# Reordering the products of a gated linear attention among GpSimd, VectorE and the schedule's slots, in a fused attention, low-rank mix and two-FFN kernel

## The chip, the cores and the metric

The kernel runs on one core of a Trainium2 chip. The time is that of one execution on the device, in microseconds (us); lower is better. All operands are float32; matmul operands of the feed-forward parts are split into a rounded part ("hi") and a remainder ("lo").

## The reference

The input has 4 batches, 8 heads, 768 tokens and head size 48.

```
f = sigmoid(f_logit)                       # attention with a gated state
state = f[t][:, None] * state + outer(k[t], v[t])
y[t] = q[t] @ state
x = y, heads side by side                  # 4 x 768 x 384
u = x + (x.T @ U @ V).T                    # low-rank mix over tokens, rank 32
x = u + relu(u @ w_ch1) @ w_ch2            # 384 -> 1536 -> 384
h = relu(x @ w_in)                         # 384 -> 1024
c = 3-tap convolution of h over tokens, by channel
out = (h * sigmoid(c)) @ w_out             # 1024 -> 384
```

## The kernel before

**Work.** Tokens go in units of 128; two units are a duo, so a batch is 3 duos and the whole input is duos 0 to 11 (`NDUO`). The attention of a duo is a list of steps (`STEPS`): `EVEN`, levels 0 to 5, `T`, `U`, `Y`. Within chunks of 64 tokens the products of gates are built by doubling. `EVEN` makes each token's own product of q and k (`blocks<-q_t,k_t`, L1031), multiplies the even tokens of q by their gates on VectorE (L1034) and then those of k on GpSimd (L1187, `k_t<-k_t,gates`), after which GpSimd makes the products of pairs of gates (L1190). At a level TensorE makes 64 small matmuls of q and k (L595). Then VectorE multiplies half of q by the gate products (L1041 at level 0, L1052 above), copies the scores that belong to the level from PSUM under a mask (`take_scores`, L988 and L994), and from level 2 on makes the products for the next level (`blocks<-blocks`, L1059, "the merge"); GpSimd multiplies half of k (L1187, `k_t<-k_t,blocks`) and at level 1 also makes the next products (L1190). The next level's matmuls wait for q, for k and for the scores taken. `T` transposes k on TensorE (L605), `U` updates the states (L617, with L1011 to L1022 on VectorE), `Y` makes the output y (L641).

**Feed-forward.** After attention a batch has a low-rank sum (`rank`: L679 on TensorE, L1085 and L1088 on VectorE), its split in three parts of 32 rows in `rstack` (`rank_split`: three ScalarE copies L882, one VectorE subtraction L1093) and the mix (L690, L697). Then come 24 slots of the first feed-forward part (`first1`, L712 to L714; `second1`, L731 to L736, two slots later) and 16 slots of the second (`first2`, L751 to L753; `second2`, L770 to L775, three slots later). In a slot q of `first2` ScalarE applies the relu (L916), VectorE makes the convolution in three instructions (L1131 and two L1134), ScalarE the sigmoid (L903), VectorE the product with h (`mul2`, L1118), ScalarE the rounded part (L909) and GpSimd the remainder (`lo2`, L1224). The convolution of slot q writes one of two buffers and waits for `lo2` of slot q - 2. At `x2_split` GpSimd makes a remainder of the input of the second part (L1218).

**Order.** One list, `ORDER`, made by `schedule()`, holds all tasks; each engine runs its own part of each task in that order, in its own queue, and waits on semaphores. Duos 0 to 2 run ahead of all feed-forward work. The steps of duos 3(b+1) to 3(b+1)+2 are laid into the slots of batch b: slot numbers go from 0 to 39, with one level per slot in `first1` and one in two slots in `first2`. In each slot the order is: in batch 0 two weight pieces (`piece`: a load issued by SyncE, a rounding copy by ScalarE L875, a remainder by GpSimd L1197), the first matmuls, the attention step, the second matmuls, `whole`, `x2_split` (GpSimd), `second2`, `split2` (which holds `lo2` of the slot before).

The step `EVEN` of a batch's first duo stands in slot 0 of the batch in which it runs, and that of the others one slot before level 0.

Of the kernel before, what the change touches and what calls it, by code (L numbers as in the profile page):

```python
# [68 lines left out]
def schedule():  # L69
# [17 lines left out]
    for b in range(B):  # L87
# [5 lines left out]
        if b + 1 < B:  # L93
            n = DUOS * (b + 1)
            for j in range(DUOS):
                for i, st in enumerate(STEPS):
                    s = (len(STEPS) + 1) * j + i + (st == Y and j < DUOS - 1)
                    if b == 0:
                        s -= 2
                        if s < 0:  # L100
                            continue

                    s = s if s < 2 * N1 else 2 * s - 2 * N1
                    at.setdefault(s, []).append((n + j, st))
        left = list(range(FIRST + 3, len(PIECES))) if b == 0 else []
        for s in range(2 * N1 + 2 * N2):
            if s < 2 * N1:
                order += [("piece", left.pop(0)) for _ in range(2) if left]
                order.append(("first1", b, s))
                if s < 2:  # L110
                    order += [("mix", b, CT + i) for i in ([0], [1, 2])[s]]
            else:
                order += [("states", n) for n, st in at.get(s - 1, []) if st == U]
                order.append(("first2", b, s - 2 * N1))
            if s < 2 * N1:
                order += [("states", n) for n, st in at.get(s - 1, []) if st == U]
            for n, st in at.get(s, []):
                order.append(("att", n, st))
                if st == U and n + 1 < NDUO:
                    order.append(("gates", n + 1))  # L120
            q = s - LAG1
            if 0 <= q < 2 * N1:
                order.append(("second1", b, q))
                if q % N1 == N1 - 1:
                    order.append(("x2", b, q // N1))
            if s in WHOLE_SLOTS:
                order.append(("whole", b, WHOLE_SLOTS.index(s)))
            for part in range(2):
                i = s - LAG1 - N1 * (part + 1)
                if 0 <= i < CT:  # L130
                    order.append(("x2_split", b, part, i))
            q = s - 2 * N1 - LAG2
            if b + 1 < B and s == 2 * N1 + 2 * N2 - 1:
                order += [("rank", b + 1, j) for j in range(DUOS)]
            if q >= 0:
                order.append(("second2", b, q))
                if q % N2 == N2 - 1:
                    order.append(("out", b, q // N2))
            if s > 2 * N1:
                order.append(("split2", b, s - 2 * N1 - 1))  # L140
# [47 lines left out]
def taken(n, st):  # L188

    return TAKEN_AT["att", n, st]  # L190
# [117 lines left out]
def bass_gla_lowrank_mix_ffn_gated_conv_ffn(nc, qT, kT, fT, qn, kn, vn, vp, mix_u, mix_v, w_ch1, w_ch2,  # L308
                                            w_in, conv_w, w_out, mask_in, ident_in, out):
    with ExitStack() as ctx:  # L310
# [83 lines left out]
        carried, y_done = sem("carried"), sem("y_done")  # L394
        x_copied, x_copied_last = sem("x_copied"), sem("x_copied_last")
        rank_done, rank_summed = sem("rank_done"), sem("rank_summed")
        rank_hi_ready, rank_ready = sem("rank_hi_ready"), sem("rank_ready")
        mix_done, u_hi_ready, u_lo_ready = sem("mix_done"), sem("u_hi_ready"), sem("u_lo_ready")
        ff1_done, r_hi_ready, r_lo_ready = sem("ff1_done"), sem("r_hi_ready"), sem("r_lo_ready")
        second_done = sem("second_done")  # L400
# [156 lines left out]
        def _(pe):  # L557
# [124 lines left out]
            def mix_task(b, i):  # L682
# [9 lines left out]
                first, width = units[0] * P, (CUT if part == 0 else HALF)  # L692
                if i == 0:
                    pe.wait_ge(rank_ready, b + 1)
                    pe.wait_ge(rank_hi_ready, 3 * (b + 1))
                    pe.wait_ge(vstack_ready, 1)
                pe.matmul(o[:, 0:width], rstack[:, t * P:(t + 1) * P], vstack[:, first:first + width],  # L697
                          start=False, stop=True, skip_group_check=True).then_inc(mix_done, 1)
# [99 lines left out]
        def _(act):  # L798
# [78 lines left out]
            def rank_split(b):  # L877
                act.wait_ge(rank_summed, 3 * (b + 1))
                if b > 0:
                    act.wait_ge(mix_done, 2 * CT * b)  # L880
                for i in (2, 0, 1):
                    nc.scalar.copy(rstack[RANK * i:RANK * (i + 1), :], rank_sum[:]).then_inc(rank_hi_ready, 1)  # L882

            def mix_task(b, i):
# [77 lines left out]
        def _(dve):  # L962
# [61 lines left out]
            def attention(n, st):  # L1024
# [21 lines left out]
                elif st < LEVELS:  # L1046
# [4 lines left out]
                    view = split_blocks(q, c)[:, :, 1, :]  # L1051
                    nc.vector.tensor_tensor(view, view, block_product(products(gates[i], blocks[i], st), c, 0),  # L1052
                                            ALU.mult).then_inc(q_ready, 1)
                    if by_vector(n, st):
                        dve.wait_ge(level_taken, taken(n, st - 1))
                        take_scores(n, st)
                    if st >= 2:
                        pairs = products(gates[i], blocks[i], st).rearrange("p (n two) -> p n two", two=2)
                        nc.vector.tensor_tensor(products(gates[i], blocks[i], st + 1), pairs[:, :, 0], pairs[:, :, 1],  # L1059
                                                ALU.mult).then_inc(merged_ready, 1)  # L1060
                elif st == T and n == 0:
                    dve.wait_ge(vstack_hi, 1)
                    lo = slice(RANK, 2 * RANK)
# [13 lines left out]
            def rank_task(b, j):  # L1077
# [2 lines left out]
                dve.wait_ge(rank_done, UNITS * (b + 1))  # L1080
                if b > 0:
                    dve.wait_ge(rank_ready, b)
                    dve.wait_ge(rank_hi_ready, 3 * b)
                sums = [ring_bank(ring_use(b, "rank", 0), DM)[RANK * i:RANK * (i + 1), :] for i in range(3)]
                nc.vector.tensor_copy(rank_sum[:], sums[0]).then_inc(rank_summed, 1)  # L1085
                for i in (1, 2):
# [1 line left out]
                    nc.vector.tensor_tensor(rank_sum[:], sums[i], rank_sum[:], ALU.add).then_inc(rank_summed, 1)  # L1088

            def rank_split(b):  # L1090
                dve.wait_ge(rank_hi_ready, 3 * b + 1)
                lo = slice(2 * RANK, 3 * RANK)
                nc.vector.tensor_tensor(rstack[lo, :], rank_sum[:], rstack[lo, :], ALU.subtract).then_inc(rank_ready, 1)  # L1093

# [69 lines left out]
        def _(pool):  # L1164
# [5 lines left out]
            def attention(n, st):  # L1170
# [9 lines left out]

                    pool.wait_ge(q_ready, scaled(n, EVEN))
                else:
                    pool.wait_ge(level_done, levels(n, st))
                    pool.wait_ge(k_ready, gated(n, st - 1))
                    products_made(pool, n, st)
                view = split_blocks(k, c)[:, :, 0, :]
# [102 lines left out]
```

## Time and profile before

| what | value |
|---|---|
| time, median of 3 runs | 724.39 us (724.3 to 727.32) |
| time of the profiled execution | 722.35 us |
| its span in the profile | 720.5 us |
| TensorE matmul busy | 683.1 us, 95% |
| VectorE busy | 430.1 us, 60% |
| GpSimd busy | 282.6 us, 39% |
| ScalarE busy | 251.0 us, 35% |

The span is what the trace covers; the profiled execution's own time is 1.85 us longer. A busy share is the union of an engine's instruction times over the span, and an instruction's time includes what it spends held up once it has started. PE is the matmul side of TensorE, DVE is VectorE, ACT ScalarE, POOL GpSimd.

### The profile page before, as it was taken

The numbers are of one execution on the slowest core, as the hardware profiler recorded it, in microseconds if no ns is written. First come the engines' busy times: TensorE is split into PE (matmuls) and PEld (weight loads), VectorE is DVE, ScalarE is ACT, GpSimd is POOL, SyncE is SP. The second block draws the span as 40 slices with busy tenths as digits, with TensorE's granted clock in tenths as the row PEclk, the third lists the DMA queues.
The fourth block names the chain that finished last, engine by engine and source line by source line (L and its number), as shares of the span: only waits on it lengthen the run. The fifth ranks groups of instructions, "written<-read, shape, count | busy, mean of one in ns | idle before, by whom it ended". The sixth has DMA issues, their size and how long they took to land.

```text
span 720.5 us, 22499 instructions
## 1 busy us (share of the span) xinstructions
PE 683.1 (95%) x10076; PEld 644.5 (89%) x10076; DVE 430.1 (60%) x721; ACT 251.0 (35%) x512; POOL 282.6 (39%) x262
## 2 busy tenths in 40 slices
PE   2897899999999999999999999999999999999998
PEld 1786788998999989999999889989999989999997
DVE  6895753754787664364597765265389751122875
ACT  1044534251255512113245431312144551121553
POOL 4872774883442243152263235045154221030432
PEclk9999999999999999999999999999999999999999
DMA  8331544322002010200201110211000100000000
GB/s 206 92 92 37 146 135 115 95 78 67 3 23 79 26 32 24 61 9 25 67 2 56 46 57 3 59 32 25 24 2 2 35 34 1 0 1 1 1 34 33
DMA packets 22720, 33.47 MB, mean 46 GB/s; under 512 B 3584, under 2 KB 15616, under 8 KB 22624
## 3 DMA queue, kind: packets, MB, share of 16 engines
q1 hardware_dynamic: 21616, 30.27, 15.0%
q10 hardware_dynamic: 1008, 1.77, 1.0%
q8 instruction: 79, 1.29, 0.8%
q14 instruction: 17, 0.14, 0.1%
HBM read 27.31 MB, written 4.72 MB: 44 GB/s over the span
## 4 chain that ended last, share of the span: by engine, by line
PE 86%; DVE 5%; POOL 4%; issue 3%; ACT 2%; DMA 1%; ACTq 0%; DVEq 0%; POOLq 0%
PE acc L731 8%; PE att L595 8%; PE acc L732 7%; PE acc L736 6%; PE hb L712 6%; PE hb L713 6%; PE hb L714 6%; PE acc L770 5%; PE hb L751 5%; PE hb L753 5%; PE hb L752 5%; PE acc L771 5%; PE acc L775 5%; PE att L641 3%; POOL k_t L1187 3%
## 5 line engine op out<-in xcount | busy, mean ns | idle before, releaser
L1104 DVE SCALAR_TENSOR_TENSOR r_lo<-hb,r_hi 128x386 fp32r<-128x386 f32 (+1 forms) x96 | 53.5, 558 | 195.3 <-ACT r_hi L894 195.2
L894 ACT ACTIVATE r_hi<-hb 128x386 fp32r<-128x386 f32 (+1 forms) x96 | 47.2, 492 | 256.5 <-PE hb L714 256.5
L1224 POOL TENSOR_TENSOR r_lo<-conv,r_hi 128x384 fp32r<-128x384 f32 x64 | 63.7, 995 | 147.3 <-ACT r_hi L909 147.3
L1187 POOL TENSOR_TENSOR k_t<-k_t,blocks 112x512 f32<-112x512 f32 x60 | 81.7, 1364 | 89.9 <-PE att L595 81.0
L731 PE MATMUL acc<-r_hi,w_ch_hi 128*128 128x386 f32 (+1 forms) x288 | 103.1, 358 | 0.0
L712 PE MATMUL hb<-u_hi,w_ch_hi 128*128 128x386 f32 (+1 forms) x288 | 98.2, 341 | 0.2 <-DVE r_lo L1104 0.2
L713 PE MATMUL hb<-u_hi,w_ch_lo 128*128 128x386 f32 (+1 forms) x288 | 97.6, 339 | 0.0
L732 PE MATMUL acc<-r_hi,w_ch_lo 128*128 128x386 f32 (+1 forms) x288 | 97.3, 338 | 0.0
L714 PE MATMUL hb<-u_lo,w_ch_hi 128*128 128x386 f32 (+1 forms) x288 | 96.9, 337 | 0.0
L595 PEld LDWEIGHTS att<-q_t,k_t 48*64 48x64 f32 (+3 forms) x3840 | 58.7, 134 | 28.9 <-issue 16.8
L1134 DVE SCALAR_TENSOR_TENSOR conv<-hb,convw,conv 128x384 f32<-128x384 f32 x128 | 79.1, 618 | 4.5
L595 PE MATMUL att<-q_t,k_t 48*64 48x32 f32 (+3 forms) x3840 | 65.3, 219 | 12.2 <-POOL k_t L1187 6.9
L1187 POOL TENSOR_TENSOR k_t<-k_t,gates 112x512 f32<-112x512 f32 x12 | 18.4, 1536 | 123.6 <-DVE q_t L1034 123.6
L770 PE MATMUL acc<-w_out_hi,r_hi 128*128 128x384 f32 x192 | 66.6, 347 | 0.0
L736 PE MATMUL acc<-r_lo,w_ch_hi 128*128 128x386 f32 (+1 forms) x288 | 66.0, 337 | 0.0
L751 PE MATMUL hb<-u_hi,w_in_hi 128*128 128x388 f32 x192 | 65.4, 341 | 0.0
L753 PE MATMUL hb<-u_lo,w_in_hi 128*128 128x388 f32 x192 | 65.0, 338 | 0.0
L752 PE MATMUL hb<-u_hi,w_in_lo 128*128 128x388 f32 x192 | 64.8, 338 | 0.0
L771 PE MATMUL acc<-w_out_lo,r_hi 128*128 128x384 f32 x192 | 64.7, 337 | 0.0
L1052 DVE TENSOR_TENSOR q_t<-q_t,blocks 112x512 f32<-112x512 f32 x60 | 60.1, 1002 | 4.1 <-PE att L595 2.4
L903 ACT ACTIVATE conv<-conv 128x384 f32<-128x384 f32 x64 | 33.7, 526 | 77.1 <-DVE conv L1134 77.1
L731 PEld LDWEIGHTS acc<-r_hi,w_ch_hi 128*128 128x128 f32 x288 | 54.2, 188 | 2.2
(140 smaller groups left out, 1295.9 us busy)
## 6 DMA issues: line engine op xcount, KB each, us to landing
v_p<-in_vn_dram SPq DMA_DIRECT2D x12, 384.0 KB, 3.6
out_dram<-ostage SPq DMA_DIRECT2D x24, 192.0 KB, 2.1
q_t<-in_qT_dram SPq DMA_DIRECT2D x21, 192.0 KB, 3.5
k_t<-in_kT_dram SPq DMA_DIRECT2D x21, 192.0 KB, 3.3
gates<-in_fT_dram SPq DMA_DIRECT2D x21, 192.0 KB, 3.5
ostage<-in_w_ch_dram SPq DMA_DIRECT2D x14, 192.0 KB, 2.9
conv<-in_w_ch_dram SPq DMA_DIRECT2D x10, 192.0 KB, 2.8
ostage<-in_w_out_dram SPq DMA_DIRECT2D x5, 192.0 KB, 2.5
```

The lines of the kernel that those rows point to most:

```text
L595: mm = pe.matmul(banks[o:o + left, par, g * C + half:g * C + half + 32], k[rows, first:first + left], moving, start=True, stop=True, skip_ ...
L712: pe.matmul(o, wh[:, t, ws], u_hi[:, t, cols], start=(t == 0), stop=False)
L713: pe.matmul(o, wl[:, t, ws], u_hi[:, t, cols], start=False, stop=False)
L714: mm = pe.matmul(o, wh[:, t, ws], u_lo[:, t, cols], start=False, stop=(t == CT - 1))
L731: pe.matmul(o, wh[:, j, ws], r_hi[:, s, 0:width], start=(j == 0), stop=False)
L732: pe.matmul(o, wl[:, j, ws], r_hi[:, s, 0:width], start=False, stop=False)
L736: mm = pe.matmul(o, wh[:, j, ws], r_lo[:, s, 0:width], start=False, stop=(j == N1 - 1))
L751: pe.matmul(o, wh[:, t, ws], u_hi[:, t, cols], start=(t == 0), stop=False)
L752: pe.matmul(o, wl[:, t, ws], u_hi[:, t, cols], start=False, stop=False)
L753: mm = pe.matmul(o, wh[:, t, ws], u_lo[:, t, cols], start=False, stop=(t == CT - 1))
L770: pe.matmul(o, r_hi[:, s, ts], wh[:, j, :], start=(j == 0), stop=False)
L1187: nc.gpsimd.tensor_tensor(view, view, block_product(ends, c, 1), ALU.mult).then_inc(k_ready, 1)
```

## The change

The edit has five parts.

1. GpSimd's product of k at a level no longer waits for the level's matmuls alone. At level 1 it waits for VectorE's product of q of this level, and at levels 2 to 5 for VectorE's merge.
2. On VectorE the merge goes ahead of the masked copy.
3. The step `EVEN` of a duo goes one slot earlier, next to `Y` of the duo before; that of the first duos of batches 2 and 3 (duos 6 and 9) goes from slot 0 of the batch in which it ran to slot 38 of the one before. Duo 3's stays.
4. The two weight pieces of a slot go from ahead of the first matmuls to behind the attention step.
5. In the split of the low-rank sum the middle rows are copied by VectorE instead of ScalarE, with a semaphore of their own.

```diff
@@ schedule() @@
-                    s = (len(STEPS) + 1) * j + i + (st == Y and j < DUOS - 1)
+                    s = (len(STEPS) + 1) * j + i + (st == Y and j < DUOS - 1) - (st == EVEN)
                     if b == 0:
                         s -= 2
-                        if s < 0:
-                            continue
+                    if s < 0:
+                        continue
...
+            if b + 2 < B:
+                at.setdefault(2 * N1 + 2 * N2 - 2, []).append((n + DUOS, EVEN))
         left = list(range(FIRST + 3, len(PIECES))) if b == 0 else []
         for s in range(2 * N1 + 2 * N2):
             if s < 2 * N1:
-                order += [("piece", left.pop(0)) for _ in range(2) if left]
                 order.append(("first1", b, s))
...
                     order.append(("gates", n + 1))
+            order += [("piece", left.pop(0)) for _ in range(2) if left]
             q = s - LAG1
@@ scalar, rank_split @@
-                for i in (2, 0, 1):
+                for i in (2, 0):
                     nc.scalar.copy(rstack[RANK * i:RANK * (i + 1), :], rank_sum[:]).then_inc(rank_hi_ready, 1)
@@ vector, attention, levels 1 to 5 @@
-                    if by_vector(n, st):
-                        dve.wait_ge(level_taken, taken(n, st - 1))
-                        take_scores(n, st)
                     if st >= 2:
                         pairs = products(gates[i], blocks[i], st).rearrange("p (n two) -> p n two", two=2)
                         nc.vector.tensor_tensor(products(gates[i], blocks[i], st + 1), pairs[:, :, 0], pairs[:, :, 1],
                                                 ALU.mult).then_inc(merged_ready, 1)
+                    if by_vector(n, st):
+                        dve.wait_ge(level_taken, taken(n, st - 1))
+                        take_scores(n, st)
@@ vector, rank_split @@
-                dve.wait_ge(rank_hi_ready, 3 * b + 1)
+                dve.wait_ge(rank_summed, 3 * b + 3)
+                if b > 0:
+                    dve.wait_ge(mix_done, 2 * CT * b)
+                nc.vector.tensor_copy(rstack[RANK:2 * RANK, :], rank_sum[:]).then_inc(rank_mid_ready, 1)
+                dve.wait_ge(rank_hi_ready, 2 * b + 1)
@@ gpsimd, attention @@
-                    pool.wait_ge(level_done, levels(n, st))
+                    if st == 1:
+                        pool.wait_ge(q_ready, scaled(n, st))
+                    else:
+                        pool.wait_ge(merged_ready, merged(n, st))
                     pool.wait_ge(k_ready, gated(n, st - 1))
```

The waits of TensorE's mix and of VectorE's rank sum on `rank_hi_ready` are split in two to match.

## Rows read from the trace of the kernel before

**Rows 1.** windows: us, busy us and count of each engine, granted clock, DMA share, GB/s

```profile
76.00:80.00 4.00, 2.58 (x12) 2.46 (x12) 3.32 (x5) 3.58 (x8) 2.06 (x3) 0.67 0.39 81
245.00:415.00 170.00, 167.61 (x2525) 157.27 (x2524) 103.95 (x178) 57.73 (x116) 58.71 (x52) 1.00 0.13 37
```

**Rows 2.** waits of PE, 80 to 585 us: us in total, times, longest

```profile
PE att L595 <- POOL k_t L1187: 4.3, 8, 1.0
```

**Rows 3.** timeline, 252 to 257 and 276 to 278 us: start, duration, engine, line, operation, idle before

```profile
252.97 0.68 DVE L1031 TENSOR_TENSOR blocks<-q_t,k_t 112x512 f32<-112x512 f32 x1
...
254.53 1.50 POOL L1187 TENSOR_TENSOR k_t<-k_t,gates 112x512 f32<-112x512 f32 x1 [6.94 <-DVE q_t L1034]
...
255.99 1.04 POOL L1190 TENSOR_TENSOR blocks<-gates 112x512 f32<-112x512 f32 x1
...
256.08 1.14 PE L595 MATMUL att<-q_t,k_t 48*64 48x32 f32 x64 [0.93 <-POOL k_t L1187]
...
276.87 0.76 PE L595 MATMUL att<-q_t,k_t 48*32 48x32 f32 x64
```

**Rows 4.** source view of L1187: count, duration min/median/max in ns

```profile
L1187 POOL TENSOR_TENSOR k_t<-k_t,blocks x60: 1049/1224/1837, 21.6 to 552.2; 112x512 f32<-112x512 f32 x60
L1187 POOL TENSOR_TENSOR k_t<-k_t,gates x12: 1487/1504/1877, 11.7 to 516.9; 112x512 f32<-112x512 f32 x12
```

**Rows 5.** costliest groups of the page, L1052: busy us, mean ns, idle before

```profile
L1052 DVE TENSOR_TENSOR q_t<-q_t,blocks 112x512 f32<-112x512 f32 x60 | 60.1, 1002 | 4.1 <-PE att L595 2.4
```

**Rows 6.** timeline, 87 to 92.5 us

```profile
86.44 1.97 POOL L1197 TENSOR_TENSOR w_ch_lo<-ostage,w_ch_hi 128x384 fp32r<-128x384 f32 x2
...
87.91 3.12 DVE L1052 TENSOR_TENSOR q_t<-q_t,blocks 112x512 f32<-112x512 f32 x1
...
91.80 0.91 PE L595 MATMUL att<-q_t,k_t 48*56 48x32 f32 x54 [2.18 <-DVE scores L994]
```

**Rows 7.** timeline of the start, before 78 us

```profile
13.23 1.94 PE L595 MATMUL att<-q_t,k_t 48*64 48x32 f32 x64 [1.80 <-POOL k_t L1187]
...
55.62 0.69 DVE L1052 TENSOR_TENSOR q_t<-q_t,blocks 112x512 f32<-112x512 f32 x1
...
56.41 1.08 PE L595 MATMUL hb<-q_t,k_t 48*32 48x32 f32 x64 [1.59 <-DVE q_t L1052]
...
75.74 1.58 ACT L882 CAST rstack<-rank_sum 32x384 fp32r<-32x384 f32 x3 [2.71 <-DVE rank_sum L1088]
...
77.42 0.66 PE L697 MATMUL hb<-vstack,rstack 96*128 96x386 f32 x1 [1.42 <-DVE rstack L1093]
```

**Rows 8.** timelines of DVE, POOL and PE, 352 to 400 us

```profile
364.30 0.79 DVE L1052 TENSOR_TENSOR q_t<-q_t,blocks 112x512 f32<-112x512 f32 x1
...
369.87 1.01 POOL L1218 TENSOR_TENSOR u_lo<-ostage,u_hi 128x382 fp32r<-128x382 f32 x1 [0.42 <-ACT u_hi L899]
...
382.02 0.76 PE L595 MATMUL att<-q_t,k_t 48*32 48x32 f32 x64
...
389.15 0.93 PE L605 MATMUL att<-ident_r,k_t 112*128 112x112 f32 x8
```

**Rows 9.** timelines of DVE and PE, ends of the first and second batch

```profile
238.21 1.27 DVE L1134 SCALAR_TENSOR_TENSOR conv<-hb,convw,conv 128x384 f32<-128x384 f32 x2
240.07 0.56 DVE L1118 TENSOR_TENSOR conv<-hb,conv 128x384 f32<-128x384 f32 x1 [0.59 <-ACT conv L903]
240.71 0.62 DVE L1131 TENSOR_SCALAR conv<-hb,convw 128x384 f32<-128x384 f32 x1
...
242.55 0.54 DVE L1085 COPY rank_sum<-hb 32x384 f32<-32x384 f32 x1
...
246.63 0.42 PE L697 MATMUL hb<-vstack,rstack 96*128 96x386 f32 x1
...
405.64 1.27 DVE L1134 SCALAR_TENSOR_TENSOR conv<-hb,convw,conv 128x384 f32<-128x384 f32 x2
...
415.99 0.42 PE L697 MATMUL hb<-vstack,rstack 96*128 96x386 f32 x1
```

More of the change, by code:

```diff
@@ L396, in bass_gla_lowrank_mix_ffn_gated_conv_ffn @@
         rank_done, rank_summed = sem("rank_done"), sem("rank_summed")
-        rank_hi_ready, rank_ready = sem("rank_hi_ready"), sem("rank_ready")
+        rank_hi_ready, rank_mid_ready, rank_ready = sem("rank_hi_ready"), sem("rank_mid_ready"), sem("rank_ready")
         mix_done, u_hi_ready, u_lo_ready = sem("mix_done"), sem("u_hi_ready"), sem("u_lo_ready")
@@ L694, in mix_task @@
                     pe.wait_ge(rank_ready, b + 1)
-                    pe.wait_ge(rank_hi_ready, 3 * (b + 1))
+                    pe.wait_ge(rank_hi_ready, 2 * (b + 1))
+                    pe.wait_ge(rank_mid_ready, b + 1)
                     pe.wait_ge(vstack_ready, 1)
@@ L1082, in rank_task @@
                     dve.wait_ge(rank_ready, b)
-                    dve.wait_ge(rank_hi_ready, 3 * b)
+                    dve.wait_ge(rank_hi_ready, 2 * b)
+                    dve.wait_ge(rank_mid_ready, b)
                 sums = [ring_bank(ring_use(b, "rank", 0), DM)[RANK * i:RANK * (i + 1), :] for i in range(3)]
```

## The prediction

> **What bounds the kernel.** I read the page's busy shares first, then the waits of PE, then the windows by stage and the timelines around each part of the edit. Behind the start TensorE is the bound: from 245 to 415 us, one batch's period, its matmuls are busy 167.6 of 170 us, while VectorE is busy 104 and GpSimd 59 [rows 1]. So time on VectorE or GpSimd is worth something only where it ends in a wait of PE. Between 80 and 585 us PE waits eight times for `k_t` of L1187, 4.3 us in all [rows 2]. These are the eight duos 4 to 11: `EVEN` sits one slot before level 0, and the chain L1031, q by gates, k by gates ends too late. The reader sees one in [rows 3]: L1031 starts at 252.97, GpSimd's product at 254.53, 1.56 later, and PE, idle for 0.93 us, starts level 0 at 256.08.
>
> In the start (duos 0 to 2, no feed-forward work to cover anything) the engines wait for each other. VectorE's and GpSimd's products also hold each other up: L1052 takes 0.69 us in [rows 7] but 3.12 in [rows 6], and 1.00 on average over 60 [rows 5].
>
> **Part 3, gains.** With `EVEN` a slot earlier the chain ends before PE comes to level 0, so the eight waits go: **-4.2 us** (4.3 less a remainder) [rows 2]. Its instructions are the same, and it passes no DMA. In `first1` the 1.4 us on VectorE and 2.5 on GpSimd that come a slot earlier are hidden by PE's two slots of lag; uncovered they would cost 2.5 a duo.
>
> **Part 3, slot 38.** Here it costs. GpSimd's queue now holds, for duos 6 and 9, k by gates (1.5 us, never under 1.487 [rows 4]), the pair products (1.04 [rows 3]) and only then `lo2` of slot 13 (1.0, as L1218 of the same width [rows 8]). The first waits for VectorE, which comes to `EVEN` only behind the convolution of slot 14; and the convolution of slot 15 waits for that `lo2`, with the rank sum, the split and the mix behind it. First batch: the convolution of slot 14 ends at 239.5 [rows 9]. Then 1.56 to GpSimd's start [rows 3], 1.5, 1.04 and 1.0 give 244.6 for the start of the convolution of slot 15, against 240.71 now [rows 9]. A convolution is 1.84 (240.71 to 242.55), so the rank sum starts at 246.4. Three instructions of 0.54, one ScalarE copy of 0.53 [rows 7] and the subtraction (0.54 too) end at 249.1. PE's L697 starts at 246.63 today with nothing to wait for; it would start at about 249.2: **+2.6 us**. Second batch: the convolution of slot 14 ends at 406.9, so that of slot 15 starts at 412.0, the rank sum at 413.8, L697 at 416.6 instead of 415.99: **+0.7** [rows 9]. Both +3.3, bounded below by 0 (if PE is later by then for other reasons and VectorE is not) and above by 5.2 (both like the first).
>
> **Parts 1 and 2.** A level's product of k (1.05 us when free [rows 4]) starts today at once when the level is done; now it waits for q (0.69 [rows 7]) and the merge. The merge alone is not in my rows; it has 128 to 16 columns against 512 in L1052, so by that row's 0.69 I take 0.2 (bounds 0.1 and 0.69). In `first1` PE goes from level 0 to level 5, five slots, in 20.8 us (256.08 to 276.9), 4.2 a slot [rows 3]; the level takes 1.14 and k is ready some 2.0 after it, so that 1 us is left: hidden. In `first2` it isn't, since VectorE comes to the level only behind the slot's convolution, and GpSimd keeps `x2_split` and `lo2` queued behind k. The loop is: convolution ends, q 0.69, merge 0.2, handing over 0.1, k 1.05, `x2_split` 1.0 and `lo2` 1.0 [rows 8], convolution of the next slot 1.84, sigmoid and `mul2` 1.1 (239.5 to the end of the row at 240.07), convolution 1.84: 8.8 us for two slots, 7.8 without `x2_split`. PE needs 7.1 for two slots (382.02 to 389.15 [rows 8]). Batches 1 and 2 begin it at 364.3: two rounds bring the convolution before level 5 to its end at 381.9, k to 383.9; VectorE's instructions overlap their successors by some 0.08, which makes it 383.4. PE wants it at 382.02: 1.3 to 1.9 late. One more round gives k of level 5 at 391.2 to 391.7 against PE's transpose at 389.15 plus the delay so far: 0.6 to 0.9 more. **+2.0 us** each for the second and third batch. In the first batch duo 5 is one level ahead and only one round with `x2_split` precedes the transpose; the same sum gives **+0.65**. Together +4.65; bounds 0 (a merge of 0.1 and a handover of nothing save 0.2 a round, not enough; only if VectorE reaches the level sooner than in the row) and 9 (each merge 0.69).
>
> **Part 1 in the start.** Here k follows q and merge on a VectorE that is 3 duos deep. GpSimd's k no longer fights q, so q saves what k loses: until about 50 us I find the levels within 0.3 us of today, following the queue. Then VectorE's first state updates stand between the levels of duo 2: q starts at 55.62 and PE's last level at 56.41 waits for it [rows 7], k being long done. Now k follows: 0.69, 0.2, 0.1 and 1.05 from 55.7 give 57.7: **+1.3 us**. Bounds -2 (q's blocked time comes back) and +4.
>
> **Part 4.** In batch 0, q at 87.91 needs 3.12 us since GpSimd goes through two pieces, k and another piece, and PE waits 2.18 [rows 6]. Now GpSimd stops ahead of k at the end of the first two pieces, 88.4: q 89.1, merge 89.3, k 90.45, PE at 90.5 instead of 91.80: **-1.3 us**, bounds 0 and -2.2. The loads and ScalarE's copies move with the pieces, on SP behind the loads of the step: TensorE needs the pieces two or more slots after their place, which hides it; each slot missed would cost up to 1.
>
> **Part 5.** Three ScalarE copies take 1.58 us and PE starts 0.1 after them [rows 7]; two take 1.06. VectorE's new copy (at most 0.54, as L1085 [rows 9]) ends before the first of them: **-0.5 us** once; at later batches PE is not waiting there.
>
> **Sum.** -4.2 + 3.3 + 4.65 + 1.3 - 1.3 - 0.5 = +3.25, so 722.35 becomes 725.6 for the profiled execution. That one is 2.04 below the median of the runs, which gives **727.6, say 727.5**.
>
> **The skill.** q at 87.91 took 3.12 us instead of 0.69 while GpSimd worked [rows 6]. The Trainium skill, "SBUF — State Buffer", section "Who interferes with whom", says that a VectorE instruction with two SBUF inputs and a GpSimd instruction that reads SBUF exclude each other for the whole instruction, and the trace agrees. By that rule, separating them in time gives back what they block; this is rival C.
>
> **The rivals.** I call the forecast A.
> A, all of the above, 0.60, own range 725 to 731.
> B, the loop in `first2` stays ahead of PE: +4.65 becomes 0 and the time 723. For it: PE is never seen waiting there today. Against it: 8.8 against 7.1 us. 0.13.
> C, faster: the blocked time comes back and PE sees no new wait. L1052 lost 60 x (1.00 - 0.69) = 19 us [rows 5]; where VectorE isn't the bound it's worth nothing, but it would make each level's q and scores earlier, cover the late k in the start, and bring VectorE early to `EVEN` in slot 38. Then -4.2 - 1.3 - 0.5 and 0 for the rest: 718.5. It decides if the convolution of slot 15 begins before some 241.8, so that its rank sum ends by PE's L697. Against it: GpSimd's 1.5 + 1.04 + 1.0 lie in that path whatever VectorE does. 0.15.
> D, slower through TensorE's clock: a level of 64 matmuls takes 1.94 us at 13.23 and 1.14 at 256.08 [rows 3, 7], the lower level of 1.2 GHz against 2.4, and 76 to 80 us shows a mean granted clock of 0.67 [rows 1]. If the later k moves the rise behind the 3.2 us of `Y` of duo 0 and the stretch at 0.67 doubles, that adds 1.6 + 1.7: 731. 0.12. The Trainium skill, "TensorE: Matmul & The Clock Gate", section "HAM oscillation — how this bites in real kernels", says that waits of TensorE can throw it back to the lower clock; the trace agrees in that PE had just waited 1.42 us at 77.42 [rows 7].
>
> **How the numbers follow.** 0.5%, or 3.6 us, is about what this kernel's measurement can tell. Slower by more (over 728.0): of A 0.33, of D 0.11, so 0.44. Faster by more (under 720.8): C 0.15, of B 0.04, of A 0.02: 0.21. The rest, 0.35. The range of 8 in 10 leaves out half of C below and the upper ends of A and D: 719.5 to 732; A's own stands above.
>
> **What would show it.** In the changed profile: no PE wait for `k_t` before level 0 of duos 4 to 11 (else part 3 failed); the L1131 of slot 15 about 4 us later against its `mul2`, and PE idle ahead of L697 at the ends of batches 0 and 1, but not 2; PE waits for L1187 at levels 5 and T in `first2`, with L1131 released by L1224; L882 with two copies and PE there 0.5 earlier; L1052 near 0.69 nearly everywhere. It is wrong if GpSimd's `EVEN` in slot 38 starts ahead of the end of the convolution, or if k follows the level by under 2 us in `first2`.

## The result and the profile after

The changed kernel takes 734.12 us, median of 4 runs (731.12 to 736.08), against 724.93 us for the kernel before, run beside it. The ratio is 1.0112, with a 95% interval of 1.0087 to 1.0138: about 8.1 us slower (the two medians are 9.2 us apart; the gains and losses in time below go by the ratios). Forecast were 727.5 us and a range that ends at 732. The direction was right, the size was not, and the time lies outside the range. The profiled execution took 734.93 us, with a span of 733.1.

Both kernels were later profiled once more, unchanged ("second pair" of profiles: before 723.76 us, span 721.9; after 731.09 us, span 729.3). The spans of that pair are 7.4 us apart, those of the first 12.6. In one experiment, e5, the profiled execution had a mean granted clock of 0.862 (span 763.5 us), so only its other nine runs are used.

The busy times, from the page of the kernel after:

```profile
PE 688.2 (94%) x10076; PEld 647.5 (88%) x10076; DVE 402.7 (55%) x725; ACT 247.6 (34%) x508; POOL 260.7 (36%) x262
```

VectorE lost 27 us of busy time and GpSimd 22, for about the same work. The two engines hold each other up less (VectorE's product of q takes 0.76 us on average instead of 1.00), and the kernel is slower all the same: TensorE bounds it, and it has new waits. These are PE's waits from 80 to 600 us in the kernel after (total, times, longest; lines have moved by 2 to 12), which answer to [rows 2]:

```profile
PE att L597 <- POOL k_t L1199: 4.4, 5, 1.2
PE hb L700 <- DVE rstack L1101: 3.6, 3, 1.9
PE acc L773 <- ACT ostage L933: 1.8, 2, 0.9
PE att L643 <- DVE state L1025: 1.7, 3, 0.6
PE att L607 <- POOL k_t L1199: 1.2, 3, 0.5
PE hb L715 <- POOL w_ch_lo L1209: 0.9, 1, 0.9
PE att L597 <- DVE scores L991: 0.8, 2, 0.4
PE acc L778 <- POOL r_lo L1236: 0.7, 1, 0.7
```

The first row looks like the one of before, 4.3 us in 8 waits. It is a different set: the eight waits ahead of level 0 are gone, and the five that stand here belong to one level of the first part in batch 0 and to levels 4 and 5 in the second part.

**Second feed-forward part of batch 1**, kernel after, timeline of all engines, which answers to [rows 8]:

```profile
379.24 0.68 DVE L1055 TENSOR_TENSOR q_t<-q_t,blocks 112x512 f32<-112x512 f32 x1
379.84 0.22 DVE L1059 TENSOR_TENSOR blocks<-blocks 112x64 f32<-112x64 f32 x1
380.14 1.11 POOL L1199 TENSOR_TENSOR k_t<-k_t,blocks 112x512 f32<-112x512 f32 x1 [3.81 <-DVE blocks L1059]
381.20 1.00 POOL L1230 TENSOR_TENSOR u_lo<-ostage,u_hi 128x382 fp32r<-128x382 f32 x1
382.17 1.83 POOL L1236 TENSOR_TENSOR r_lo<-conv,r_hi 128x384 fp32r<-128x384 f32 x2
383.06 0.62 DVE L1139 TENSOR_SCALAR conv<-hb,convw 128x384 f32<-128x384 f32 x1 [1.93 <-POOL r_lo L1236]
...
387.88 0.68 DVE L1055 TENSOR_TENSOR q_t<-q_t,blocks 112x512 f32<-112x512 f32 x1
...
389.87 0.76 PE L597 MATMUL att<-q_t,k_t 48*32 48x32 f32 x64 [1.12 <-POOL k_t L1199]
...
397.59 0.99 PE L607 MATMUL att<-ident_r,k_t 112*128 112x112 f32 x8 [0.46 <-POOL k_t L1199]
...
400.48 0.53 ACT L906 ACTIVATE conv<-conv 128x384 f32<-128x384 f32 x1 [3.07 <-DVE conv L1142]
...
402.02 1.24 ACT L933 COPY ostage<-acc 128x384 f32<-128x384 f32 x3
...
402.63 0.41 PE L773 MATMUL acc<-w_out_hi,r_hi 128*128 128x384 f32 x1 [0.89 <-ACT ostage L933]
```

The reader sees the loop close: q, merge, k, `x2_split`, `lo2`, and only then the convolution, which had waited 1.93 us for `lo2`. From one q to the next are 8.64 us (379.24 to 387.88). The last four rows show what the loop leads to: ScalarE's sigmoid (L906) waits 3.07 us for the late convolution, the copy of the finished output (L933) stands behind it in ScalarE's queue, and TensorE needs the bank that this copy empties. In the kernel before, the copy ran 0.5 us after the matmuls, and PE never waited for it:

```profile
391.42 1.24 ACT L930 COPY ostage<-acc 128x384 f32<-128x384 f32 x3 [0.49 <-PE acc L775]
```

**End of batch 0**, kernel after, timeline, which answers to [rows 9]:

```profile
242.38 1.27 DVE L1142 SCALAR_TENSOR_TENSOR conv<-hb,convw,conv 128x384 f32<-128x384 f32 x2
...
245.15 1.52 POOL L1199 TENSOR_TENSOR k_t<-k_t,gates 112x512 f32<-112x512 f32 x1 [4.67 <-DVE q_t L1037]
...
246.63 1.04 POOL L1202 TENSOR_TENSOR blocks<-gates 112x512 f32<-112x512 f32 x1
...
247.63 1.83 POOL L1236 TENSOR_TENSOR r_lo<-conv,r_hi 128x384 fp32r<-128x384 f32 x2
248.53 0.62 DVE L1139 TENSOR_SCALAR conv<-hb,convw 128x384 f32<-128x384 f32 x1 [2.99 <-POOL r_lo L1236]
...
248.55 0.79 PE L778 MATMUL acc<-w_out_hi,r_lo 128*128 128x384 f32 x3 [0.69 <-POOL r_lo L1236]
...
250.37 0.54 DVE L1089 COPY rank_sum<-hb 32x384 f32<-32x384 f32 x1
...
253.25 0.45 PE L700 MATMUL hb<-vstack,rstack 96*128 96x386 f32 x1 [1.90 <-DVE rstack L1101]
```

GpSimd starts `EVEN`'s k 1.50 us after the convolution of slot 14 has ended (243.65), `lo2` follows behind 1.52 and 1.04, VectorE stands idle 2.99, and PE waits twice, 0.69 and 1.90. Behind this wait the clock fell in this execution. A window of the kernel after (busy time and count of PE, PEld, DVE, ACT and POOL, then the granted clock, 0.55, and DMA):

```profile
254.00:256.00 2.00, 2.00 (x11) 1.92 (x11) 1.03 (x2) 1.20 (x3) 1.00 (x1) 0.55 0.00 0
```

**Where the time goes.** I take the start of one group of matmuls in both kernels and see how far the one of after lies behind. The table gives what each stretch adds. T is the transpose L607 of a duo, "rank" the first L681 at the end of a batch, "mix" the first L700 behind it. The forecast column sorts the terms of the prediction into the same stretches, 0.5 for each wait of `EVEN`.

| stretch | first pair | second pair | forecast |
|---|---|---|---|
| start to first mix matmul | +4.55 | +0.89 | +0.8 |
| to last mix matmul of batch 0 | -0.54 | -0.53 | 0 |
| to T of duo 3 | -1.13 | -1.14 | -1.3 |
| to T of duo 4 (one `EVEN` wait) | -0.80 | -0.79 | -0.5 |
| to rank (one `EVEN` wait, second part of batch 0) | +1.44 | +1.42 | +0.1 |
| rank to mix (slot 38) | +3.10 | +3.13 | +2.6 |
| to T of duo 7 (two `EVEN` waits) | +0.15 | -1.44 | -1.05 |
| to rank (one, second part of batch 1) | +2.85 | +2.89 | +1.5 |
| rank to mix (slot 38) | +1.59 | +1.60 | +0.7 |
| to T of duo 10 (two) | -1.45 | -1.48 | -1.05 |
| to rank (one, second part of batch 2) | +2.88 | +2.83 | +1.5 |
| sum | +12.6 | +7.4 | +3.3 |

The second pair is the one to read: behind 82 us neither of its traces shows a lower granted clock. (The second row holds two things that cancel in part: the lower clock that both traces of before have at 77 to 82 us, and a new wait of 0.93 for a weight piece.) The first pair has two surpluses over it, 3.7 us in the start, where the kernel after has a granted clock of 0.50 from 74 to 80 us, and 1.6 behind the clock's fall at 254 us.

### The profile page after: what moved, and what is told of

Same layout as the page of the kernel before. It is cut to its first block, busy times and chain, and to the rows that moved or that the text cites. A ratio compares the mean times of both kernels' runs of the same rounds, so it can differ in the third digit from the quotient of the medians.

```text
span 733.1 us, 22509 instructions
## 1 busy us (share of the span) xinstructions
PE 688.2 (94%) x10076; PEld 647.5 (88%) x10076; DVE 402.7 (55%) x725; ACT 247.6 (34%) x508; POOL 260.7 (36%) x262
## 4 chain that ended last, share of the span: by engine, by line
PE 63%; DVE 14%; POOL 4%; issue 3%; ACT 3%; ACTq 0%; DVEq 0%
PE acc L734 8%; PE acc L735 7%; PE acc L739 7%; PE hb L715 6%; PE hb L716 6%; PE hb L717 6%; PE att L597 5%; DVE conv L1142 5%; DVE conv L1139 3%; PE att L643 2%; PE acc L773 2%; POOL k_t L1199 2%; PE acc L774 2%; PE hb L754 2%; PE hb L756 2%
## 5 line engine op out<-in xcount | busy, mean ns | idle before, releaser
L1199 POOL TENSOR_TENSOR k_t<-k_t,blocks 112x512 f32<-112x512 f32 x60 | 69.0, 1149 | 202.0 <-DVE blocks L1059 117.6
L1236 POOL TENSOR_TENSOR r_lo<-conv,r_hi 128x384 fp32r<-128x384 f32 x64 | 61.4, 965 | 111.3 <-ACT r_hi L912 111.3
L715 PE MATMUL hb<-u_hi,w_ch_hi 128*128 128x386 f32 (+1 forms) x288 | 98.0, 340 | 1.1 <-POOL w_ch_lo L1209 0.9
L597 PE MATMUL att<-q_t,k_t 48*64 48x32 f32 (+3 forms) x3840 | 64.8, 219 | 10.6 <-POOL k_t L1199 7.5
L906 ACT ACTIVATE conv<-conv 128x384 f32<-128x384 f32 x64 | 33.7, 527 | 102.2 <-DVE conv L1142 102.2
L755 PE MATMUL hb<-u_hi,w_in_lo 128*128 128x388 f32 x192 | 64.8, 338 | 0.0
L1139 DVE TENSOR_SCALAR conv<-hb,convw 128x384 f32<-128x384 f32 x64 | 39.2, 612 | 35.6 <-POOL r_lo L1236 24.6
L715 PEld LDWEIGHTS hb<-u_hi,w_ch_hi 128*128 128x128 f32 x288 | 54.2, 188 | 1.7 <-DVE u_lo L1107 1.2
```

The costliest lines, as they stand in the source:

```text
L597: mm = pe.matmul(banks[o:o + left, par, g * C + half:g * C + half + 32], k[rows, first:first + left], moving, start=True, stop=True, skip_ ...
L715: pe.matmul(o, wh[:, t, ws], u_hi[:, t, cols], start=(t == 0), stop=False)
L1199: nc.gpsimd.tensor_tensor(view, view, block_product(ends, c, 1), ALU.mult).then_inc(k_ready, 1)
```

## The experiments

Each kernel but the last two was timed beside the kernel before, and its ratio is to that; what changes between two kernels is read from their ratios, since the kernel before took 725 to 727 us from one set of runs to the next. Theory Q of the expectations is the forecast's: the loop in the second part and slot 38 cost TensorE waits. Its rivals put the loss into the start and TensorE's clock, or into the merge ahead of the masked copy.

**e1_no_slot38.** The changed kernel, `EVEN` of duos 6 and 9 back in slot 0.

```diff
-                    s = (...) - (st == EVEN)
+                    s = (...) - (st == EVEN and j > 0)
...
-            if b + 2 < B:
-                at.setdefault(2 * N1 + 2 * N2 - 2, []).append((n + DUOS, EVEN))
```

> The changed kernel with EVEN of duos 6 and 9 back in slot 0 of their own batch; all else as changed. Theory Q (queue order: in slot 38 GpSimd's products stand ahead of the remainder that the next convolution waits for): the waits ahead of the mix at the ends of batches 0 and 1 go, the fall of the clock behind the first goes too, and two waits for k before level 0 of about 1.1 us come back: 4 to 5 us faster than the changed kernel, some 729.5. Rival F (the loss is nearly all in the loop of the second feed-forward part and in the start): within 1.5 us of the changed kernel.

Measured: 728.77 us, ratio 1.0050 (1.0030 to 1.0071). From 1.0112 that is 0.0062, or 4.5 us, net of the two waits ahead of level 0 (0.93 and 0.96 in its trace), which are back. The offset doesn't move between rank and mix of batch 0 (1.89 to 1.90), where the changed kernel adds 3.1. The place and the sign of this term are shown. The expectation that the fall of the clock would go was wrong: it fell here too, at 258 us, behind the wait of 0.93.

**e2_k_free and e3_k_free_merge_back.** In e2 GpSimd's k waits for the level alone; the merge stays ahead. In e3 VectorE's order is that of before too. Parts 3, 4, 5 and slot 38 stay in both.

```diff
-                    if st == 1:
-                        pool.wait_ge(q_ready, scaled(n, st))
-                    else:
-                        pool.wait_ge(merged_ready, merged(n, st))
+                    pool.wait_ge(level_done, levels(n, st))
```

> The changed kernel, but GpSimd's product of k waits for the level's matmuls again, as before the change; the merge stays ahead of the masked copy. Theory Q: the waits for k at levels 4, 5 and T in the second feed-forward part go, and with them those for the states and for the stored output behind them: 8 us of stalls, and 1 to 3 in the start: 724 to 726. Rival M (the merge ahead of the masked copy is what delays the next level, by the scores): 731 or more, with waits of PE for the scores. Rival K (most of the start's loss is TensorE's clock, whatever k waits for): not under 726.

> As e2_k_free, and the merge is behind the masked copy again, so that parts 1 and 2 of the change are undone whole. Theory Q: within 1 us of e2_k_free, since the merge is short and PE doesn't wait for the scores. Rival M: 5 us or more below e2_k_free.

Measured: e2 728.23 us, ratio 1.0034 (1.0010 to 1.0057); e3 725.97 us, ratio 1.0009 (0.9991 to 1.0026). In both the loss of the second part is gone (the offset changes there by -0.66 and 0.02 in batches 1 and 2 of e2, by -0.65 and -0.69 in e3, where an `EVEN` wait went), while waits of 1.90 and 0.4 us at mix stay, against 1.90 and 1.35 in the changed kernel. So k's new wait makes the one and slot 38 the other. e2 is over the 724 to 726 us that theory Q gave it, and e3, expected within 1 us of e2, is 1.8 below it by the ratios. e2 also shows what that same wait is good for. The timeline of e2 in batch 0:

```profile
89.84 3.12 DVE L1055 TENSOR_TENSOR q_t<-q_t,blocks 112x512 f32<-112x512 f32 x1
90.28 1.17 POOL L1196 TENSOR_TENSOR k_t<-k_t,blocks 112x512 f32<-112x512 f32 x1
91.40 2.41 POOL L1206 TENSOR_TENSOR w_ch_lo<-ostage,w_ch_hi 128x384 fp32r<-128x384 f32 x2
92.88 1.08 DVE L1059 TENSOR_TENSOR blocks<-blocks 112x128 f32<-112x128 f32 x1
...
94.70 1.53 PE L597 MATMUL att<-q_t,k_t 48*56 48x32 f32 x56 [3.17 <-DVE scores L997]
```

GpSimd's k and two pieces run back to back, VectorE's q takes 3.12 us instead of 0.68, and TensorE waits 3.17 us; in e3 it waits 2.17, in the changed kernel 1.06. Behind these waits the granted clock fell to 0.50 and 0.62 from 94 to 98 us, in the changed kernel it did not. The merge ahead costs 1.8 us by the two ratios, which the intervals don't part from nothing. The traces do show a price where k is free: PE's waits for scores (L997) are 3.17, 1.33 and 0.59 us in e2, and 2.17, 0.56 and none in e3, 2.4 us less.

**e4_parts_3_4_5.** The kernel before with `EVEN` earlier for the second and third duo of a batch, the pieces behind the attention step and the rank split. No slot 38, parts 1 and 2 left out.

> The kernel before with EVEN one slot earlier for the second and third duo of a batch only (nothing in slot 38), with the weight pieces behind the attention step and with the split of the rank sum shared. Theory Q: six waits of 0.6 to 0.7 us before level 0 go (3.9 us), 0.5 for the rank sum and up to 1 for the pieces: 719 to 721, faster than both kernels. Rival: moving EVEN earlier costs elsewhere what it gives (a wait for the states, seen at 0.6 us): 724.

Measured: 722.37 us, ratio 0.9958 (0.9938 to 0.9978). The offset falls by 0.54 at the split of the first low-rank sum, and the waits ahead of level 0 of these duos are gone. But the wait in batch 0 stands as in [rows 6], 2.19 us for scores, with q at 3.14 us: moving the pieces alone does not help there. The expected 719 to 721 us was missed by a little.

**e5_free_in_second_ff and e6_free_in_start.** The changed kernel with k waiting for the level alone in the third duos (e5), or in duos 0 to 2 (e6).

```diff
-                    if st == 1:
+                    if n in (5, 8, 11):        # e6: if n < DUOS
+                        pool.wait_ge(level_done, levels(n, st))
+                    elif st == 1:
```

> The changed kernel, but for duos 5, 8 and 11, whose levels lie in the second feed-forward part, GpSimd's product of k waits for the level's matmuls again. Theory Q (the loop of convolution, k and remainder is slower than TensorE there): the changed kernel's profile loses 1.4 us in that stretch of batch 0 and 3.5 in each of batches 1 and 2, 8.4 in all, so about 726. Rival S (parts 1 and 2 cost mainly in the start): 731 or more.

> The changed kernel, but for duos 0 to 2 GpSimd's product of k waits for the level's matmuls again. Theory Q: k behind q and merge costs 1 to 2 us there: 732 to 733. Rival C (what the start lost is TensorE's clock, which rose 6 us later in the changed kernel's profile because TensorE waited for k more often): 729 to 731. Rival N (the rise varies from run to run whatever the kernel): 734, as the changed kernel.

Measured: e5 722.72 us, ratio 0.9962 (0.9934 to 0.9989); e6 732.21 us, ratio 1.0076 (1.0047 to 1.0105). e5 gives back 0.0150, 10.9 us, from a wait in three duos: most of the loss is k's wait in the second part. e6 gives back 2.6 us, and its interval overlaps that of the changed kernel. This rules the start out as the main place; the waits in e6's second part are those of the changed kernel. e5 came out faster than the 726 us expected. Between theories Q and C of e6 the runs don't decide: its 732.21 us lies in Q's range, but the kernel before took 727.0 beside it.

**e7_remainder_first and e8_k_behind_q.** Both are e4 with one thing more. In e7 `EVEN` of duos 6 and 9 goes to slot 38, but behind `split2`, which holds `lo2`. In e8 k waits for q in duos 3 and 4 alone.

```diff
             if s > 2 * N1:
                 order.append(("split2", b, s - 2 * N1 - 1))
+            if b + 2 < B and s == 2 * N1 + 2 * N2 - 2:        # e7
+                order.append(("att", DUOS * (b + 2), EVEN))
...
-                    pool.wait_ge(level_done, levels(n, st))
+                    if n in (3, 4):                           # e8
+                        pool.wait_ge(q_ready, scaled(n, st))
+                    else:
+                        pool.wait_ge(level_done, levels(n, st))
```

> The kernel of parts 3, 4 and 5 (e4), with EVEN of duos 6 and 9 in slot 38 as in the change, but in GpSimd's queue behind the remainder of slot 13. Theory Q: it is the place in GpSimd's queue that costs, not the slot. VectorE's two products fit before its convolution of slot 15 at no cost to TensorE, and the two waits before level 0 of 0.93 and 0.96 us go: 1 to 2 us faster than e4, some 721. Rival: VectorE's 1.4 us delay the rank sum and the mix by as much: no faster than e4, 722.4 or more.

> e4, with GpSimd's product of k behind VectorE's of q for duos 3 and 4 alone (no wait for the merge). Theory L (GpSimd's back-to-back instructions keep VectorE out until its queue stops): q of duo 3 at level 2 takes some 0.7 to 1.2 instead of 3.14 us and PE's wait of 2.19 us falls to about 1: 1.1 faster than e4, some 721.3. Rival: the pieces alone keep VectorE out as long: no change.

Measured: e7 722.17 us, ratio 0.9923 (0.9893 to 0.9954); e8 720.60 us, ratio 0.9901 (0.9871 to 0.9932). In e7 nothing waits at either mix and both waits of duos 6 and 9 are gone: slot 38 was no bad place, only the order in it. That is seen best against e3, which differs from e7 in nothing but `EVEN`'s place within slot 38, ahead of `lo2` there, behind it here: 1.0009 against 0.9923, 6.2 us, clear of the intervals. First e3, then e7, timelines of PE at the end of batch 0:

```profile
254.94 0.45 PE L700 MATMUL hb<-vstack,rstack 96*128 96x386 f32 x1 [1.90 <-DVE rstack L1101]
```

```profile
248.69 0.42 PE L700 MATMUL hb<-vstack,rstack 96*128 96x386 f32 x1
```

From rank to mix e3 adds 2.42 and 0.62 us in batches 0 and 1, e7 nothing; the timed difference is larger than these 3.0, and how much of the rest is the clock stays open: in the profiles the granted clock of e3 fell behind its wait, that of e7 did not. Against e4, e7 gains 2.5 us by the ratios, whose intervals overlap.

e8 takes the gain of part 1 without its price. The timeline of e8 in batch 0:

```profile
87.11 1.27 DVE L1053 TENSOR_TENSOR q_t<-q_t,blocks 112x512 f32<-112x512 f32 x1
...
88.46 1.15 POOL L1197 TENSOR_TENSOR k_t<-k_t,blocks 112x512 f32<-112x512 f32 x1 [0.63 <-DVE q_t L1053]
...
89.66 1.03 PE L595 MATMUL att<-q_t,k_t 48*56 48x32 f32 x64 [0.85 <-POOL k_t L1197]
```

q takes 1.27 us instead of 3.14 in e4, and PE waits 0.85 instead of 2.19. From the last mix matmul of batch 0 to T of duo 3, e8 gains 1.33 us on the kernel before, and e7, whose k is that of e4 and whose clock stays up there, 0.03.

**e9_best and e10_mended.** e9 is e7 and e8 in one. e10 is the changed kernel with the two repairs: k free in duos 5, 8 and 11, and `EVEN` behind `lo2` in slot 38.

> This is the kernel before with parts 3, 4 and 5, EVEN of duos 6 and 9 in slot 38 but behind the remainder of the slot, no merge ahead of the masked copy, and k behind q in duos 3 and 4 alone: e7 and e8 together. Theory 1 (prices add where each removes a wait of TensorE): e7's ratio was 0.9923 and e8's 0.9901, and e7 took over e4 (0.9958) about 2.5 us in its profile where the two k waits before level 0 at the batch ends went. Added to e8's 716.0 us span that gives a span of about 714.5 and a ratio of 0.987; TensorE's wait ahead of the first level of batch 0 is 0.85 as in e8, and no wait for k stands at the batch boundaries. Rival (the two gains are the same time: a granted clock that stayed high): ratio 0.990 to 0.992, equal to e8 or e7.

> This is the changed kernel with two repairs: in duos 5, 8 and 11 k waits for the level alone, and EVEN of duos 6 and 9 stands in slot 38 behind the remainder. Theory (the second feed-forward part and slot 38 are where the loss sits): the waits of TensorE for k, of the second products for stored output and of the mix for the split (1.90 and 1.35 us) all go; from e5's 0.9962 this takes another 3 to 5 us, 719 to 721 us and a ratio of 0.989 to 0.992. What is left against the kernel before is then the start alone. Rival (the merge ahead of the copy, which stays everywhere here, costs by itself): the ratio stays at e5's 0.996 or above, with waits for scores taken of about 2 us in the first feed-forward part.

Measured: e9 716.42 us, ratio 0.9862 (0.9833 to 0.9891); e10 719.12 us, ratio 0.9904 (0.9874 to 0.9934). The two repairs turn a loss of 1.1% into a gain of 1.0%. PE's waits in e10, 80 to 600 us:

```profile
PE att L643 <- DVE state L1025: 1.2, 2, 0.6
PE att L597 <- POOL k_t L1201: 1.1, 1, 1.1
PE hb L700 <- DVE rstack L1101: 0.9, 1, 0.9
PE hb L715 <- POOL w_ch_lo L1211: 0.9, 1, 0.9
PE att L597 <- DVE scores L991: 0.8, 2, 0.4
```

The wait for `ostage` is gone with those for k in the second part, although nothing was done about it: it was their consequence. The 0.9 for the split is that of batch 0. The merge is still ahead of the copy, and no wait of 2 us for scores appears, so here it is not what costs. Against the second profile of the changed kernel, e10 loses 8.5 us less in the three stretches with a second part (1.4, 3.6 and 3.5). e9 is faster than either kernel of this case. That the gains of e7 and e8 add (0.987 expected, 0.9862 measured) fits with each having removed waits of its own; the interval leaves out the rival's 0.990 to 0.992, if narrowly.

**e11_before_again and e12_after_again.** Both kernels once more.

> The kernel before, unchanged, looked at once more. Theory 1 (where the granted clock rises in the start, and the short low stretch behind it, is set by the order of the instructions): the rise comes at 60.3 us again and the low stretch at 77.4 to 80.8. Theory 2 (it varies from execution to execution): it comes elsewhere, by several us, as it did among kernels whose start was the same up to 50 us (60.2 to 62.2 with the start of before, 66.6 to 78.6 with that of after).

> The changed kernel, unchanged, looked at once more. Theory 1 (set by the order of the instructions): the clock rises at 66.6 us again, is low at 73.4 to 80.3 and at 254.3 to 257.8. Theory 2 (it varies by execution): the rise lies anywhere between 62 and 79. The waits for k in the second feed-forward part, and the 1.90 and 1.35 us before the mix, repeat within 0.1 us under either.

Measured: 723.76 and 731.09 us. Behind the start e12 repeats the waits within 0.1 us (4.4 and 1.3 for k, 1.8 for `ostage`), but not the clock; the wait at the first mix, 0.35 us in the first profile, is 0.88. Its L700 at the end of batch 0 waits just as long, and the granted clock stays at 1.00 behind it. The timeline of e12, and a window of it:

```profile
250.99 0.44 PE L700 MATMUL hb<-vstack,rstack 96*128 96x386 f32 x1 [1.90 <-DVE rstack L1101]
```

```profile
254.00:256.00 2.00, 2.00 (x13) 1.98 (x12) 0.13 (x1) 1.24 (x3) 0.00 (x0) 1.00 0.15 55
```

In the start the rise to 2.4 GHz varies as well, and with the same instructions. It is read from the duration of the matmuls: the granted clock of the windows from 60 to 70 us is 1.00 in all traces, also where matmuls take the time of the lower level. The same 64 matmuls in the first and in the second profile of the kernel after:

```profile
62.94 1.96 PE L643 MATMUL att<-v_p,scores 64*64 64x48 f32 x64
```

```profile
63.12 1.15 PE L643 MATMUL att<-v_p,scores 64*64 64x48 f32 x64
```

e8 and e9 have the same order up to slot 38 of batch 0. First e8, then e9, timelines of PE:

```profile
60.86 1.15 PE L641 MATMUL att<-v_p,scores 64*64 64x48 f32 x64
...
74.60 1.08 PE L595 MATMUL att<-q_t,k_t 48*64 48x32 f32 x64
```

```profile
60.66 1.96 PE L643 MATMUL att<-v_p,scores 64*64 64x48 f32 x64
...
77.00 1.08 PE L597 MATMUL att<-q_t,k_t 48*64 48x32 f32 x64
```

Again they take 1.15 us in one and 1.96 in the other, the two levels of 2.4 and 1.2 GHz, and batch 0 begins 2.4 us later. Over all profiles but that of e5, the first group of matmuls at the higher level starts between 60.6 and 63.2 us (before twice, e1, e4, e8, second profile of after), at 67.5 (first profile of after) or not before 74 (e2, e3, e6, e7, e9, e10): both kinds of start have early and late ones. Nor is the fall behind a batch's end tied to slot 38: e8, without it, has a granted clock of 0.57 from 254 to 258 us, behind a wait of 0.93 us, behind which the clock of the kernel before stayed at 1.00. The order of the instructions alone does not set where the clock rises or falls.

## Why the prediction was right in direction and wrong in size

In short: the forecast sum was +3.25 us, and the second pair of profiles shows +7.4. The step that failed is the loop in the second part (+4.65): it was followed on VectorE and GpSimd up to k and no further, while the runs show a price on other queues too, above all on ScalarE's, whose late copy of the output costs TensorE 2.4 us. Three smaller things were missed: a wait for the states (0.7, part 3), a later end of the second part of batch 0 (0.8), and that the loop makes slot 38 dearer (1.6).

**EVEN earlier (-4.2).** Right, and worth more: the eight waits give 5.7 us, about 0.7 each instead of 0.54 (0.79, 0.81, 0.64, 0.81 and 0.67 in the second pair; those inside the second part, 0.67, 0.65 and 0.68, by e4, where k waits as in the kernel before). One cost was overlooked. PE waits for the states of duo 4 (L643 <- L1025), 0.62 us in the list of waits and 0.69 by the offset, and this wait is there in e4 as well, so it comes with part 3.

**Slot 38 (+3.3).** The chain was right step by step. Forecast were 9.7 us from the end of the convolution of slot 14 to L697; the trace has 9.60 (243.65 to 253.25). The offsets grow by 3.13 and 1.60, together 4.7. In e2 and e3, where the loop is gone and `EVEN` stands in the same place, they grow by 2.44 and 0.65, and by 2.42 and 0.62: 3.1 together, against 3.3 forecast. The other 1.6 us come from the loop of the second part: the convolution of slot 14 ends 0.11 us behind the first L681 in the changed kernel, and 0.54 ahead of its counterpart in the kernel before [rows 9] and in e2. The two terms had been taken as independent.

**The loop (+4.65).** The period was right: 8.64 and 7.75 us measured (387.88 to the q at 395.63), 8.8 and 7.8 forecast. The waits for k were right too: 0.47, 1.12 and 0.46 in batch 1, 2.05 together, against 2.0, though the first of them stands at level 4 already, where none was forecast. In batch 0 duo 5 is two levels ahead by the schedule, not one as the prediction has it; its wait for k is 0.47 against 0.65. This is the step that failed all the same, since it ended with k. The price of a late convolution was worked out for GpSimd and VectorE and never for ScalarE, whose queue holds the copies of the finished output behind the sigmoid. That adds 1.19 us in batch 1 and 1.17 in batch 2 by the offsets from T to the state updates of duos 8 and 11; in batch 0 there is no wait for the copy, and 0.2 us are added ahead of the state updates of duo 5 and 0.6 at its `Y`, where PE waits 0.5 for VectorE's state update (L643 <- L1025). e2, e3 and e10, with k free in these duos, have neither this wait nor the one for the copy. For the three stretches 3.1 were forecast with the `EVEN` waits taken off, and 7.1 came: 2.4 more for the copies, 0.8 more in batch 0, 0.7 for the states of duo 4, 0.6 more for k, less 0.5 for the larger `EVEN` waits. These 4.0 us are nearly the whole difference of 4.1 between the forecast sum and the second pair; the rest cancels (slot 38 +1.4; start, last mix, duo 3 and the other `EVEN` waits -1.4), which is luck.

**Part 1 in the start (+1.3) and the rank split (-0.5).** In the second pair the two come to +0.89 at the first mix, against +0.8 forecast. The split's -0.5 is seen in e4 (-0.54). PE's last level waits 1.81 us for k in both profiles of the changed kernel. The start scatters by 1 us and more between executions of the same order, so that the agreement is in part luck and the term of part 1 is only bounded: at the update behind that level four kernels with the changed start are 1.41 to 2.04 us behind the first profile of before, and six with the start of before -0.07 to 1.97. The means, 1.80 and 0.71, are 1.1 apart.

**Part 4 (-1.3).** Right number, wrong owner. The gain is there, but e4 and e7 have the pieces moved and do not show it (q at 3.14, PE waiting 2.19); e8 with k behind q does. Whether k behind q would do it with the pieces left in their old place no run shows. And the moved pieces cost a wait of 0.9 us at the first L715 (`w_ch_lo`), which stands in every kernel that has part 4 and which I had called hidden.

**The rivals.** B (the loop hidden) is refuted. C was wrong as a whole but right in its mechanism: where VectorE is in TensorE's way, in batch 0, separating the two engines shortens TensorE's wait by 1.34 us (e8 against e4), and the time by 4.1 us by the ratios. There the trace agrees with what the prediction took from the Trainium skill, "SBUF — State Buffer", section "Who interferes with whom". Elsewhere VectorE wasn't the bound, and 27 us of its time bought nothing. (C's own test, 241.8 for the start of the convolution of slot 15, comes to 242.0 by the terms of the slot 38 sum; nothing hangs on it.) D came closest in number (731), and was wrong in its cause. What it describes is seen in the first profile of after (rise at 67 us, low clock from 73 to 80), but the late rise occurs without the change, and the timed difference of 8.1 us stands beside 7.4 in a pair with no fall of the clock behind 82 us. The Trainium skill's rule that waits of TensorE can throw back the clock ("TensorE: Matmul & The Clock Gate", section "HAM oscillation — how this bites in real kernels") is borne out as a possibility only. The same wait of 1.90 us was followed by the fall in one execution and by none in the other.

**Open.** e5 gives back 10.9 us, where the table gives 8.4 for k's wait in the second part (7.1, with the three `EVEN` waits inside the stretches put back, 2.0, and the states of duo 4 taken off, 0.7); e10's trace, with the same repair, gives 8.5. The intervals are wide enough for the difference, and whether more is in it stays open. Of the 4.1 us between e8 and e4, 1.3 are the wait; how much of the rest is a clock that falls less often behind a shorter wait stays open. In the traces it fell behind the wait of 2.2 us or more in e2, e3 and e4, and not in e7, nor in either profile of before. e4 and e7 have the same instructions there, and from the last mix matmul of batch 0 to T of duo 3 e4, with the fall, takes 1.6 us more.

## What to carry to other kernels

When a change delays one instruction, follow the delay through every in-order queue until it meets the bounding engine again: here the delay was followed through VectorE's and GpSimd's queues, and the largest part that was missed was an output copy behind a sigmoid in ScalarE's. A wait that keeps two engines apart is worth having only where the freed engine is in the way; set it for those steps alone (duos 3 and 4 here: 4.1 us gained over e4 by the ratios, against a loss when set everywhere). And when a producer is moved to an earlier slot, the order within the slot decides: `EVEN` ahead of the remainder (e3) was 6.2 us slower than behind it (e7).

## What the runs showed of the hardware

Two kernels with the same instructions in the start (e8 and e9) had TensorE at the 2.4 GHz level from 60.9 us and not before 74 us, and batch 0 began 2.4 us later; a part of the late rise was taken back, since waits of 0.85 and 1.08 (issue) and 0.6 of 1.50 us (`k_end`) that the early one shows are missing in the late one. One and the same program, the kernel after, reached it by 63.1 us in one execution and not before 64.8 in another.

VectorE's time held up by GpSimd was worth little: 27 us less of it in the changed kernel, against one wait of TensorE shortened by 1.1 to 1.3 us. And waits of TensorE of equal length (2.2 us at 91 to 94 us, 1.90 at 251 to 253, 0.93 at 253 to 260) were followed by a fall of the granted clock in some executions and by none in others.
